# Splitting the level steps of ten chunks between two engines, and moving steps and filler matmuls in the attention prologue

## The reference

```python
for t in range(S):                                   # attention, S = 768
    state = alpha[:, :, t, :, None] * state + einsum('bhd,bhe->bhde', k[:, :, t], v[:, :, t])
    y[:, :, t] = einsum('bhd,bhde->bhe', q[:, :, t], state)
for e in range(4):                                   # experts, 3072 tokens, 384 -> 1024 -> 384
    out += p[:, e:e + 1] * (maximum(x @ w1[e], 0) @ w2[e])
g = h * clip(h + 3, 0, 6) / 6                        # h = x @ w_in, 384 -> 2048
return g @ w_out
```

## Time and profile before

| | |
|---|---|
| median of three runs | 1419.88 us |
| profiled execution | 1419.88 us, span 1418.1 us |
| PE busy | 1388.5 us (98%) |
| DVE busy | 731.3 us (52%) |
| ACT busy | 533.6 us (38%) |
| POOL busy | 837.6 us (59%) |
| start of `hidden(0)`, the end of the prologue | 80.69 us |
| granted clock of TensorE, mean | 0.996 of full speed |

### The profile page before, as it was taken

The page is one execution under the profiler, slowest core; times in us unless marked ns, Lnnn a source line. Parts: engine busy times, 40 slices in busy tenths (PEclk is TensorE's granted clock), DMA queues, the critical chain, the costliest instruction groups (busy, mean ns, idle before and its releaser), DMA issues.

```text
span 1418.1 us, 30461 instructions
## 1 busy us (share of the span) xinstructions
PE 1388.5 (98%) x11672; PEld 1140.5 (80%) x11672; DVE 731.3 (52%) x1383; ACT 533.6 (38%) x927; POOL 837.6 (59%) x870
## 2 busy tenths in 40 slices
PE   6789999999999999999999999999999999999998
PEld 5678888888888888888888888888888888888887
DVE  6977665545554555455545455555455343333343
ACT  2133333333344333344433335433334443335553
POOL 8867776565666565656665656565655444444442
PEclk9899999999999999999999999999999999999999
DMA  4333333333333433334333333443332333233330
GB/s 142 119 120 108 102 110 96 106 93 115 93 104 124 138 93 107 93 109 128 107 115 116 93 107 93 136 123 107 93 93 82 113 118 100 90 100 92 99 123 34
DMA packets 70366, 150.10 MB, mean 106 GB/s; under 512 B 9296, under 2 KB 21840, under 8 KB 70224
## 3 DMA queue, kind: packets, MB, share of 16 engines
q1 hardware_dynamic: 70224, 148.16, 34.5%
HBM read 143.36 MB, written 4.77 MB: 104 GB/s over the span
## 4 chain that ended last, share of the span: by engine, by line
PE 93%; POOL 4%; issue 1%; DVE 1%; ACT 0%; DMA 0%; DVEq 0%; POOLq 0%; ACTq 0%
PE h_bank L446 41%; PE out_banks L462 28%; PE out_third L462 14%; PE score_banks L358 4%; POOL k_lev L828 2%; PE score_banks L420 2%; PE turn_bank L398 1%; POOL decay L802 1%; PE score_banks L414 1%; PE turn_bank L386 1%; PE turn_bank L388 1%; POOL w_lo L842 1%; PE turn_bank L374 1%; POOL k_lev L818 0%; DMA alpha_q<-qa 0%
## 5 line engine op out<-in xcount | busy, mean ns | idle before, releaser
L842 POOL TENSOR_TENSOR w_lo<-w_raw,w_hi 128x768 fp32r<-128x768 f32 x288 | 547.6, 1902 | 528.2 <-ACT w_hi L745 528.0
L739 ACT ACTIVATE h_hi<-gated 128x512 fp32r<-128x512 f32 x288 | 182.2, 633 | 670.5 <-DVE gated L590 582.3
L446 PE MATMUL h_bank<-x_hi,w_hi 128*128 128x512 f32 x864 | 336.4, 389 | 1.1 <-issue 1.1
L446 PE MATMUL h_bank<-x_lo,w_hi 128*128 128x512 f32 x864 | 336.1, 389 | 0.0
L446 PE MATMUL h_bank<-x_hi,w_lo 128*128 128x512 f32 x864 | 336.0, 389 | 0.0
L590 DVE SCALAR_TENSOR_TENSOR gated<-h_bank,probs 128x512 f32<-128x512 f32 x192 | 132.7, 691 | 328.0 <-PE h_bank L446 328.0
L604 DVE TENSOR_TENSOR h_lo<-gated,h_hi 128x512 fp32r<-128x512 f32 x288 | 241.6, 839 | 57.5 <-ACT h_hi L739 57.5
L745 ACT ACTIVATE w_hi<-w_raw 128x768 fp32r<-128x768 f32 x288 | 239.1, 830 | 8.0 <-DMA w_raw<-w 8.0
L462 PE MATMUL out_banks<-h_hi,w_hi 128*128 128x512 f32 x576 | 233.0, 405 | 0.3 <-DVE x_lo L614 0.3
L462 PE MATMUL out_banks<-h_hi,w_lo 128*128 128x512 f32 x576 | 225.0, 391 | 0.0
L462 PE MATMUL out_banks<-h_lo,w_hi 128*128 128x512 f32 x576 | 224.5, 390 | 0.0
(11 more groups left out here) (75 smaller groups left out, 1279.5 us busy)
## 6 DMA issues: line engine op xcount, KB each, us to landing
w_raw<-w SPq DMA_DIRECT2D x288, 384.0 KB, 3.1
alpha_q<-qa SPq DMA_DIRECT2D x48, 256.0 KB, 3.5
k_raw<-kk SPq DMA_DIRECT2D x48, 128.0 KB, 3.5
probs<-prob_scratch SPq DMA_DIRECT2D x6, 1024.0 KB, 7.5
v_diag<-v SPq DMA_DIRECT2D x96, 48.0 KB, 2.4
out<-result SPq DMA_DIRECT2D x18, 256.0 KB, 3.9
level_sb<-level SPq DMA_DIRECT2D x1, 80.0 KB, 3.1
ident_sb<-ident SPq DMA_DIRECT2D x1, 64.0 KB, 2.8
```

The lines of the kernel that those rows point to most:

```text
L446: mm = pe.matmul(h_bank[g % 2][:, :], a, x, start=k == 0 and i == 0, stop=k == K3 - 1 and i == 2)
L739: act.activation(h_hi[:, g % DEEP, :], gated[:, g % 2, :], ACT.Copy).then_inc(hh_made, 1)
L842: pool.tensor_tensor(w_lo[:, g % RING, :], w_raw[:, g % RAW, :], w_hi[:, g % RING, :].bitcast(F32), ALU.subtract).then_inc(w_lo_made, 1)
```

## The change

The new rule `in_halves(n)` holds for chunks 0 to 9, those that are prepared in the prologue. For them each level step is split. The half that has a decay is multiplied by the engine that did the step before (DVE for queries, POOL for keys), over 128 elements in each partition in place of 256. The half that is multiplied by one is copied by ACT, with `even_q` for queries (five per chunk) and `odd_k` for keys (now six per chunk). Both halves of a level must be there before the next level can be made, so DVE and POOL now wait for ACT at each level, and ACT for them. The chunks from 10 on are scaled as before.

```diff
-                for step in range(3):
-                    scale_q(n + 2, step)
-                if not first_of_seq(n):
-                    decay_state(n)
-                next_state(n)
-                for step in range(3, Q_STEPS):
+                for step in range(Q_STEPS - 1):
                     scale_q(n + 2, step)
                 if n < 2:
                     for step in (range(5), range(5, 9))[n]:
                         normalise(step)
+                if not first_of_seq(n):
+                    decay_state(n)
+                next_state(n)
+                scale_q(n + 2, Q_STEPS - 1)
...
+            def even_q(n, l):
+
+                act.wait_ge(q_made, Q_STEPS * n + l + 1)
+                if l == 1:
+                    need(act, p_made, n - 1)
+                else:
+                    act.wait_ge(q_even_made, HALF_STEPS * n + l - 1)
+                if l == LEVELS - 1:
+                    need(act, y_made, n - 1)
+                act.activation(q_out(n, l + 1)[:, :, 0, :], q_halves(n, l)[:, :, 0, :], ACT.Copy
+                               ).then_inc(q_even_made, 1)
+
+            def halves(n, step):
+
+                if step % 2 == 0:
+                    odd_k(n, step // 2)
+                else:
+                    even_q(n, step // 2 + 1)
...
-            odd_k(0)
-            odd_k(1)
+            for n in range(2):
+                for step in range(LEVELS + HALF_STEPS):
+                    halves(n, step)
...
                 copy_k_rows(n)
-                odd_k(n + 2)
-                copy_y(n)
+                for step in range(LEVELS + HALF_STEPS):
+                    if step == 5:
+                        copy_y(n)
+                    halves(n + 2, step)
```

More of the change, by code:

```diff
@@ L50 @@
 KEEPS = LEVELS
+HALF_STEPS = LEVELS - 1
 SLAB = 256
@@ L115, in decayed, with in_halves, odd_count @@
     return n - n // SEQ_CH - (n + SEQ_CH - 1) // SEQ_CH
+def in_halves(n):
+    return n < Q_BEFORE
+def odd_count(n, l):
+    return LEVELS * n + l + 1 if in_halves(n) else LEVELS * Q_BEFORE + n - Q_BEFORE + 1
 def first_of_seq(n):
@@ L193, in build @@
         q_made, z_made, k_made = sem("q_made"), sem("z_made"), sem("k_made")
-        k_odd_made = sem("k_odd_made")
+        q_even_made, k_odd_made = sem("q_even_made"), sem("k_odd_made")
         p_made, kt_made, kv_made, y_made = sem("p_made"), sem("kt_made"), sem("kv_made"), sem("y_made")
@@ L339, in score @@
                 pe.wait_ge(in_k[n % QRING], 16 * (n // QRING + 1))
-                pe.wait_ge(k_odd_made, n + 1)
+                pe.wait_ge(k_odd_made, odd_count(n, LEVELS - 2))
+                if in_halves(n):
+                    pe.wait_ge(q_even_made, HALF_STEPS * n + LEVELS - 2)
                 pe.wait_ge(q_made, Q_STEPS * n + LEVELS)
@@ L366, in turn_k @@
                 pe.wait_ge(k_made, K_STEPS * (n + 1))
+                pe.wait_ge(k_odd_made, odd_count(n, LEVELS - 1))
                 need(pe, s_made, carried(n))
@@ L408, in attend @@
                 pe.wait_ge(q_made, Q_STEPS * (n + 1))
+                if in_halves(n):
+                    pe.wait_ge(q_even_made, HALF_STEPS * (n + 1))
                 need(pe, s_made, carried(n))
@@ L472, in _ @@
                     score(n + 1)
-                keep_warm(2)
                 carry(n)
                 attend(n)
-                keep_warm(2)
                 turn_y(n)
@@ L479, in _ @@
                     turn_k(n + 1)
-                keep_warm(2)
+                keep_warm(4)
             for g in range(SLOTS):
@@ L519, in scale_q @@
                         need(dve, p_made, n - 1)
+                    elif in_halves(n):
+                        dve.wait_ge(q_even_made, HALF_STEPS * n + l - 1)
                     if l == LEVELS - 1:
@@ L523, in scale_q @@
                     a, b = q_halves(n, l), q_out(n, l + 1)
-                    dec = decay_level(n, l)[:, :, 0:2].rearrange("p m (r x) -> p m r x", x=1)
-                    op = dve.tensor_tensor(b, a, dec.to_broadcast([P, m, 2, x]), ALU.mult)
+                    if in_halves(n):
+                        dec = decay_level(n, l)[:, :, 1:2].to_broadcast([P, m, x])
+                        op = dve.tensor_tensor(b[:, :, 1, :], a[:, :, 1, :], dec, ALU.mult)
+                    else:
+                        dec = decay_level(n, l)[:, :, 0:2].rearrange("p m (r x) -> p m r x", x=1)
+                        op = dve.tensor_tensor(b, a, dec.to_broadcast([P, m, 2, x]), ALU.mult)
                 op.then_inc(q_made, 1)
@@ L694, in _, with odd_k @@
         def _(act):
[L695 to L699, removed]
-                act.activation(b, a, ACT.Copy).then_inc(k_odd_made, 1)
+            def odd_k(n, l):
+                if l == 0:
+                    act.wait_ge(in_k[n % QRING], 16 * (n // QRING + 1))
+                    need(act, p_made, n - 1)
+                else:
+                    act.wait_ge(k_odd_made, odd_count(n, l - 1))
+                    act.wait_ge(k_made, K_STEPS * n + l)
+                if l == LEVELS - 1:
+                    need(act, kt_made, carried(n - 1))
+                a, b = (k_level(n, m).rearrange("p j (m r x) -> p (j m) r x", r=2, x=1 << l)[:, :, 1, :]
+                        for m in (l, l + 1))
+                act.activation(b, a, ACT.Copy).then_inc(k_odd_made, 1)
+            def even_q(n, l):
+                act.wait_ge(q_made, Q_STEPS * n + l + 1)
+                if l == 1:
+                    need(act, p_made, n - 1)
+                else:
+                    act.wait_ge(q_even_made, HALF_STEPS * n + l - 1)
+                if l == LEVELS - 1:
+                    need(act, y_made, n - 1)
[4 more added lines that the diff above has]
+                    odd_k(n, step // 2)
+                else:
+                    even_q(n, step // 2 + 1)
             def copy_k_rows(n):
@@ L778, in _ @@
                     if n + 2 < CHUNKS:
-                        odd_k(n + 2)
+                        odd_k(n + 2, 0)
                 if g in STATE_AT:
@@ L820, in scale_k @@
                 x, m = 1 << l, PAIRS * CH // 2 >> l
-                if l == 1:
-                    pool.wait_ge(k_odd_made, n + 1)
+                if in_halves(n) or l == 1:
+                    pool.wait_ge(k_odd_made, odd_count(n, l - 1))
                 if l == LEVELS - 1:
@@ L826, in scale_k @@
                 a, b = (k_level(n, l + o).rearrange("p j (m r x) -> p (j m) r x", r=2, x=x) for o in (0, 1))
-                dec = decay_level(n, l)[:, :, 2:4].rearrange("p m (r x) -> p m r x", x=1)
-                pool.tensor_tensor(b, a, dec.to_broadcast([P, m, 2, x]), ALU.mult).then_inc(k_made, 1)
+                if in_halves(n):
+                    dec = decay_level(n, l)[:, :, 2:3].to_broadcast([P, m, x])
+                    op = pool.tensor_tensor(b[:, :, 0, :], a[:, :, 0, :], dec, ALU.mult)
+                else:
+                    dec = decay_level(n, l)[:, :, 2:4].rearrange("p m (r x) -> p m r x", x=1)
+                    op = pool.tensor_tensor(b, a, dec.to_broadcast([P, m, 2, x]), ALU.mult)
+                op.then_inc(k_made, 1)
             def key_step(n, step):
```

## The result

Over five runs the changed kernel takes 1433.04 us (1427.98 to 1434.98), and the kernel before, in five runs beside them on the same chip, 1419.56 us (1419.45 to 1420.39). The ratio is 1.0085, with a 95% interval of 1.0061 to 1.0107. That is slower by 13.5 us; 6.0 were forecast. The five times lie in two groups, two near 1428 us and three between 1433 and 1435 us. The profiled execution took 1435.15 us, 15.3 more than the one of before, with a span of 1433.4 us, and the comparison of the rows goes by that one. It belongs to the slower group.

What follows compares the result with a forecast made beforehand. The prologue was to be bound by a 7.0 us ring through the engines' queues and PE's clock: hidden(0) 3.5 us later plus 2.5 in the first slots, 6.0 on 1419.88, gives 1425.9 us; 8-in-10 range 1418.5 to 1437.

Steps and rivals of the forecast that it cites:

- PE is full from chunk 10 on: From 200 to 1300 us PE is busy 1099.64 of 1100.00 us, untouched; the worth is hidden(0)'s start plus slot losses.
- The saving on DVE and POOL: Prologue passes: halving saves 1.1 us a chunk on each, pass 6.1 us if alone, but it turns into waiting.
- The ring through four queues: Prologue: state, PE's turn_y to attend, ACT's copy_y and query copy, DVE's sixth step, state; 7.0 us a pass.
- S(0): End of next_state(0) in the prologue: forecast 22.4 us, against 21.6 before.
- S(1): End of next_state(1): 8.4 us at half clock, 2.2, then normalise 0.8; forecast 33.8 us.
- cold pass: A prologue pass with PE at half clock: 10.6 us instead of 7.0, 3.6 more.
- 8.4 us of unbroken work: PE's work in the pass to S(1), claimed to give the full clock back for the passes to S(5).
- four passes of 7.0: Prologue passes from S(2) to S(5) at full clock, leading to 61.8 us.
- the first rival: Prologue clock stays half longer; one lost pass gives 1429.5 us, all four 1440.3; chance 0.22.
- S(6): End of next_state(6): copy_y(6) waits behind POOL's three w_lo, 9.6 us after S(5), then 2.2; 73.6 us.
- S(7): End of next_state(7): a half-clock pass without score, 7.9 us; forecast 81.5 us, against 78.4 before.
- `hidden(0)` 2.7 behind it: Prologue's end: turn_y(7) 0.7, zero matmuls 1.9, release 0.1; start at 84.2 us, 3.5 later than before.

Runs made afterwards that it cites:

- e2_fill_hole: The changed kernel with eight zero matmuls added between attend and turn_y; 1420.35 us, ratio 1.0000 to the kernel before.
- e4_state_third: The changed kernel with DVE's order as before, decay_state and next_state behind the third query step; 1414.26 us, ratio 0.9954.
- e7_order_alone: The kernel before with only DVE's new order, the state's steps behind six query steps, no halves; 1420.09 us, ratio 0.9994.
- e8_copy_y_later: The changed kernel with copy_y on ACT moved behind the query copy that DVE's step needs; 1417.02 us, ratio 0.9978.
- e1_three_pairs: The changed kernel with its zero matmuls in three pairs a pass, as before; 1436.43 us, ratio 1.0112.
- e5_wlo_last: e4_state_third with the first three w_lo behind chunk 9 on POOL; 1414.15 us, ratio 0.9949.
- e9_state_fill: e4_state_third with three more zero matmuls behind attend; 1416.02 us, ratio 0.9971.
- e3_one_group_alone: The kernel before with only its zero matmuls changed, one group of four instead of three pairs; 1420.59 us, ratio 1.0004.
- e6_state_pairs: e4_state_third with the zero matmuls in three pairs a pass, as in the kernel before; 1417.35 us, ratio 0.9976.
- e10_fill_wlo_last: e5_wlo_last with three more zero matmuls behind attend; 1415.25 us, ratio 0.9965.

## Why the prediction was right, and where it was too small

- **PE is full from chunk 10 on, the prologue alone counts.** Right: 1100.00 of 1100.00 us.
- **The saving on DVE and POOL turns into waiting.** Right in kind, but DVE's idle time ahead of its sixth query step was forecast at up to 1 us and is 3.5 to 5.0 us. The saving on DVE was put too high. A halved query step shows 0.29 us alone, and two in a row 0.76, so 0.38 each against the 0.52 of the earlier trace rows: five save 0.7 us a chunk, not 1.1. (By the 1.04 ns per column that the Trainium skill gives, "Vector Engine (DVE) Microarchitecture Reference", section 5.2, the estimate is 0.13 us a step and 0.67 for five; the trace agrees with it, at 0.14.) In the forecast nothing hung on it, since DVE was not to have the pace.
- **The ring through four queues, 4.8 + 2.2 us at full clock.** Right. e2_fill_hole has passes of 7.2 us at full clock: 4.8 from the end of one state to `copy_y`, and 2.4 from there to the end of the next. In the changed kernel the second part is 2.4 too (51.67 to 54.07), 0.2 more than forecast; `decay_state` took 0.57, not 0.35. That it takes both the order on DVE and the one on ACT is shown by e4_state_third, e7_order_alone and e8_copy_y_later.
- **S(0) at 22.4, S(1) at 33.8 in a cold pass.** Measured 22.5 and 34.0.
- **"8.4 us of unbroken work give the clock back, and four passes of 7.0 lead to 61.8."** This is the step that failed. Unbroken work of that length did not give the clock back: from 22.69 to 30.93 us, and again from 43.4 to 51.6, 63.7 to 71.9 and 74.5 to 82.7, PE worked for 8.2 us without a rest and the granted clock was 0.50 throughout. Where it did come back, at about 39 and 59 us, PE had worked for only 5 us behind a hole, and the next hole took it again. The four passes took 40.4 us (34.0 to 74.4) in place of 28. A cold pass was worked out right, 10.6 against the 10.8 measured twice; I had the number of them wrong. Two of the passes, 9.3 and 9.5, regained the clock in their last part and lost it in the hole. That is the first rival, which I gave 0.22, and against which I had held that only a hole of 3.62 us had cost the clock in the trace of before. The prediction put the other rests at up to 0.6 us. In the prologue of that trace there are longer ones that kept the clock, of up to 1.52 us (the row below), but none of 2.2, so it could not say what such a rest does. e2_fill_hole shows the cause: fill the hole, change nothing else in the order, and 12.7 us come back. In e1_three_pairs even 1.8 to 1.9 us lost it.

```profile
28.38 0.55 PE L398 MATMUL turn_bank<-v_diag,k_rows 128*64 128x96 f32 x8 [1.52 <-DVE x_lo L580]
```

- **S(6), 11.8 us behind the three `w_lo`.** Measured 11.1, but the wait was mostly covered: `attend(6)` at half clock itself ended only near 82.7, and PE's rest there was 2.89 us, not the nearly 7 forecast. In e4_state_third this pass takes 9.2 us, and in e5_wlo_last 5.9, so the wait is there; what it is worth to the total is nothing, since the same work is then late at `hidden(0)`.
- **S(7) 7.9 and `hidden(0)` 2.7 behind it.** Measured 7.7 and 2.2. Together with the steps above, `hidden(0)` is at 95.34 in place of 84.2.
- **2.5 us in the first slots.** Measured 0.65. Half clock lasts there to about 96.7 us, 1.4 us into `hidden(0)`.

The sum, in the profiled execution: 6.0 forecast, 12.4 more for the four passes, 1.2 less for the rest of the prologue and 1.9 less for the first slots, 15.3. The median is 13.5 above before. The runs of the changed kernel spread over 7.0 us, those of before over 0.9. That the clock comes back in other passes from run to run would fit, but only one execution has a trace, so this is argued and not shown. The mean granted clock of a run doesn't bear it out: it was 0.979 and 0.980 in the two runs near 1428 us, and 0.972, 0.980 and 0.981 in the three slower ones.

So the direction is right, and the ring with it. That the time stays inside the range given is partly luck: more than half of the loss comes from what I held to be a rival. Nor do the runs bear out 6.0 us for a kernel that keeps its clock in passes 2 to 5. In e2_fill_hole the matmuls run at full speed from 24 us on, so pass 1 isn't cold either: S(1) ends at 31.8 in place of 33.8, the first slots lose nothing, and the ratio is 1.0000.

## What to carry to other kernels

Before a step is moved behind one that waits for another engine, follow the wait around all queues: if it returns to its start, the queues' orders make a ring, and its length is the new pace, however short the work in it. Where TensorE is part of such a ring, count its longest unbroken rest in each turn, since rests far below the one that the old trace shows as costly may take the clock too (1.8 to 2.6 us here, against 3.62). A filler gave the clock back in a rest of 2.5 us (e2_fill_hole), but six records in a rest of 0.77 us came with 1.8 us more (e9_state_fill). Opening the ring is worth more than filling it: 1414.26 us against 1420.35. And where a change has several parts, run each alone: here the split was worth 3 us, and the order that came with it cost 19.

## What the runs showed of the hardware

- **Short rests that cost the clock.** In a pass with one hole of 2.55 us (the changed kernel) or of 1.8 to 1.9 us (e1_three_pairs) the granted clock fell to 1.2 GHz; with 0.57 us (e2_fill_hole) it stayed at 2.4 GHz. It isn't the hole's length alone: in e4_state_third it fell near 40 us beside pieces below 1 us, and in e3_one_group_alone near 44 us beside 1.15 and 1.27, while e7_order_alone kept it over 1.92 and 1.95 us and the kernel before over 1.52.
- **Unbroken work that did not bring it back.** In the changed kernel PE worked for 8.2 us without a rest in four passes and stayed at 1.2 GHz (granted clock 0.50). In the passes from 34.07 and 54.18 us full clock came after some 5 us, and in that from 85.58 us after 4.4. So the length of the work alone doesn't decide either.
- **A stall of PE named only "issue".** Within `attend(5)` PE stands for 3.2 to 4.1 us in five kernels: 3.62 before, and 3.61, 3.21, 3.86 and 4.12 in e6_state_pairs, e7_order_alone, e9_state_fill and e10_fill_wlo_last. It lies between 50 and 62 us in all of them, where large loads run. In e4_state_third it is 1.72 us and falls ahead of `score`:

```profile
56.49 0.38 PE L371 MATMUL out_banks<-alpha_q,k_raw 64*64 64x32 f32 x13 [1.72 <-issue]
```

The window of 50 to 64 us in e4_state_third, and below it in the changed kernel, which has no such stall:

```profile
50.00:64.00 14.00, 8.32 (x199) 7.25 (x191) 9.48 (x26) 5.46 (x21) 11.64 (x21) 0.77 0.65 198
```

```profile
50.00:64.00 14.00, 8.89 (x171) 7.90 (x167) 6.75 (x21) 5.84 (x23) 5.67 (x16) 0.62 0.19 50
```

Large loads alone don't make it. The kernels with the stall move 174 to 195 GB/s in that window and the changed kernel 50, but e2_fill_hole moves 208 there and e8_copy_y_later 222, and neither has a stall of that length. Where in PE's queue the loads fall may decide. Two things in the traces fit that. Kernels whose queue on PE is the same stall at the same record: the kernel before and e7_order_alone behind the twelfth of the sixteen records of `attend`, e9_state_fill and e10_fill_wlo_last behind the fifth. And in each of the five the DMA engines are 96% to 100% busy during the stall, and one packet of the DMA queue that the profile names `q8 instruction` falls in it. So PE may be waiting for its own instructions; this was not tried, and the cause is open. It may matter here: after each of these stalls the clock is at half, which would explain why a fuller PE (e6_state_pairs, e9_state_fill, e10_fill_wlo_last) gained nothing over e4_state_third. With one trace for each kernel, and that of e4_state_third from its fastest run, this is not shown.
